# Block sums by kind, and the transposes of x2 moved between outputs, at the start of the second mixture of experts

## The reference

```python
x = attention(q, k, v)              # 2 x 8 heads x 768 x 64, banded mask
...                                 # as rows: N = 1536 tokens, D = 512
# second layer: hard routing over 8 experts, with a skip
y[mask] = gate_w[mask, None] * (np.maximum(xc[mask] @ w1[e], 0.0) @ w2[e])
x2 = x + y
# third layer: every token through all 4 experts, F = 1024
p = domain_probs / (domain_probs.sum(-1, keepdims=True) + 1e-09)
for e in range(4):
    h = np.maximum(x2 @ w1[e], 0.0)
    out += p[:, e:e + 1] * (h @ w2[e])
```

## Time and profile before

| what | us |
|---|---|
| median of 3 runs | 790.16 |
| the three runs | 790.33, 777.43, 790.16 |
| the profiled execution, its own time | 778.11 |
| span of its trace | 776.4 |
| PE busy in it | 743.0 |
| first product of the third layer starts at | 267.3 |
| second step starts at | 308.5 |

### The profile page before, as it was taken

The page is one execution under the profiler, slowest core; times in us unless marked ns, Lnnn a source line. Parts: engine busy times, 40 slices in busy tenths (PEclk is TensorE's granted clock), DMA queues, the critical chain, the costliest instruction groups (busy, mean ns, idle before and its releaser), DMA issues.

```text
span 776.4 us, 11260 instructions
## 1 busy us (share of the span) xinstructions
PE 743.0 (96%) x4199; PEld 661.5 (85%) x4199; DVE 471.6 (61%) x924; ACT 329.1 (42%) x586; POOL 42.2 (5%) x86
## 2 busy tenths in 40 slices
PE   3999999699999879999999999999999999999998
PEld 2889889488888778998989989989889899898896
DVE  5766666699888587654573475275365265456442
ACT  2666566388988352521432333234144043143230
POOL 3100100110100410000000000000000000000000
PEclk9999999699999999999999999999999999999999
DMA  9569970599990530030021011002003003000112
GB/s 152 101 152 247 291 217 21 199 394 390 390 389 35 156 130 1 1 109 1 0 71 39 1 55 54 1 17 92 0 0 108 0 0 109 0 0 0 41 41 81
DMA packets 86944, 79.28 MB, mean 102 GB/s; under 512 B 50802, under 2 KB 56948, under 8 KB 86900
## 3 DMA queue, kind: packets, MB, share of 16 engines
q1 hardware_dynamic: 81540, 71.32, 29.6%
q0 software_dynamic: 1600, 5.24, 2.2%
q10 hardware_dynamic: 3760, 2.14, 0.9%
HBM read 70.30 MB, written 8.39 MB: 101 GB/s over the span
## 4 chain that ended last, share of the span: by engine, by line
PE 89%; DVE 6%; DMA 2%; issue 1%; ACT 1%; POOL 0%; DVEq 0%; SPq 0%; POOLq 0%
PE ps L1881 32%; PE ps L1858 30%; PE ps L1761 11%; PE ps L1585 3%; PE ps L1610 2%; PE ps L1609 2%; PE ps L1594 2%; PE ps L1565 2%; PE ps L1626 1%; PE ps L1618 1%; PE ps L1736 1%; DVE xs L1448 1%; DVE X L1105 1%; PE ps L1817 1%; DVE ql L1065 1%
## 5 line engine op out<-in xcount | busy, mean ns | idle before, releaser
L1858 PE MATMUL ps<-xs,w1s 128*128 128x384 f32 x1344 | 237.7, 336 | 0.0
L1881 PE MATMUL ps<-w2s,h_hi 128*128 128x512 f32 x768 | 237.1, 390 | 0.6 <-DVE X L1486 0.6
L1858 PEld LDWEIGHTS ps<-xs,w1s 128*128 128x128 f32 x1344 | 235.1, 189 | 1.3
L1881 PEld LDWEIGHTS ps<-w2s,h_hi 128*128 128x128 f32 x768 | 143.7, 188 | 30.2 <-DVE X L1486 1.0
L1881 PE MATMUL ps<-w2s,h_lo 128*128 128x512 f32 x384 | 149.7, 390 | 0.0
L1488 DVE SCALAR_TENSOR_TENSOR X<-ps,prn,X 128x512 f32<-128x512 f32 x84 | 63.1, 751 | 121.7 <-PE ps L1881 121.3
L953 ACT ACTIVATE shared<-ps 128x384 f32<-128x384 f32 x96 | 46.1, 488 | 157.5 <-PE ps L1858 157.3
L1457 DVE TENSOR_TENSOR shared<-ps,shared 128x384 f32<-128x384 f32 x96 | 53.4, 557 | 93.6 <-PE ps L1858 93.3
L1881 PEld LDWEIGHTS ps<-w2s,h_lo 128*128 128x128 f32 x384 | 72.1, 188 | 15.0
L956 ACT ACTIVATE h_hi<-shared 128x384 fp32r<-128x384 f32 x96 | 50.5, 527 | 67.7 <-DVE shared L1457 67.7
L1023 DVE TENSOR_TENSOR piece_lo<-ring,piece_hi 128x1024 fp32r<-128x1024 f32 x48 | 56.4, 1220 | 5.4 <-ACT piece_hi L775 5.4
(11 more groups left out here) (183 smaller groups left out, 798.3 us busy)
## 6 DMA issues: line engine op xcount, KB each, us to landing
ring<-in_moe_w SPq DMA_DIRECT2D x24, 1024.0 KB, 12.3
raw<-in_moe_w SPq DMA_DIRECT2D x16, 1024.0 KB, 5.1
shared<-in_moe_w SPq DMA_DIRECT2D x8, 1024.0 KB, 10.7
X<-in_k SPq DMA_DIRECT2D x16, 192.0 KB, 4.3
shared<-in_q SPq DMA_DIRECT2D x16, 192.0 KB, 4.3
X<-in_v SPq DMA_DIRECT2D x16, 192.0 KB, 3.1
x_d<-X SPq DMA_DIRECT2D x8, 384.0 KB, 3.2
X<-x_d SPq DMA_DIRECT2D x2, 1536.0 KB, 16.5
```

What stands on the lines that cost most here:

```text
L1858: mm = pe.matmul(out_, w1s[:, wp, WI[name], c, f * P:(f + 1) * P], xs[:, 3 * b:3 * b + 3, xp, XI[name], c, :], start=(not onto and x == 0 ...
L1881: mm = pe.matmul(ps[:, 6 + k % 2, :], h_, w2s[:, wp, c, :], start=(x == 0 and c == 0), stop=(x == 2 and c == 3))
```

## The change

Four things change, and what is computed stays the same.

1. **Sums by kind.** For pairs 0 to 2 the sums are split in three kinds instead of all four at once: kind 0 is s3 (for P7), kind 1 is s1 and s2 (for P5 and P6), kind 2 is s4 (for P3). Each kind has a semaphore of its own for the high and the low part, and each product waits for its own kind.
2. **Order of the products.** P4 comes ahead of P6, in all 16 steps. ACT and DVE take the items in the new places (`copy(8, ...)`, `add(6, ...)`), in the same order as before.
3. **Transposes of pairs 3 to 5.** None is left among the products. Pair 3, 4 and 5 are transposed behind the outputs of tiles 0, 1 and 2, in other banks, and the DVE work on them is spread between the outputs.
4. **w2 of the first unit.** `w2_high` and `w2_low` move from the first step to the front, ahead of the work on pair 0. ACT waits there for `x2_begun`, which PE sets when it has transposed the first tile.

```diff
-        PAIR_BANK = ((4, 1), (5, 2), (6, 7), (6, 7), (1, 2), (4, 5))
+        PAIR_BANK = ((4, 1), (5, 2), (6, 7), (1, 4), (2, 5), (1, 4))
+        KIND = ((5, 6), (3, 5), (6, 7))
+        KIND_OF = {"P7": 0, "P6": 1, "P5": 1, "P3": 2}
-        ITEMS = [(p, f) for p in ("P1", "P2", "P7", "P6", "P4", "P5", "P3") for f in range(2)]
+        ITEMS = [(p, f) for p in ("P1", "P2", "P7", "P4", "P6", "P5", "P3") for f in range(2)]
...
+            def kind_high(g, p):
+                i, j = KIND[g]
+                if g < 2:
+                    act.wait_ge(s_step, 3 * p + (1, 3)[g])
+                else:
+                    act.wait_ge(s_made, p + 1)
+                act.activation(xs[:, p, 0, i:j, :, :].rearrange("p a k c -> p (a k c)"),
+                               xs_f[:, p, 1, i:j, :].rearrange("p a c -> p (a c)"), ACT.Copy).then_inc(kind_hi[g], 1)
...
                 for f in range(2):
                     copy(0, 0, f)
+                if begin:
+                    for f in range(2):
+                        copy(4, 1, f)
...
-                if inserted:
-                    inserted()
-                for f in range(2):
-                    copy(4, 1, f)
+                if begin:
+                    kind_high(2, 1)
+                    kind_high(2, 2)
+                else:
+                    for f in range(2):
+                        copy(4, 1, f)
...
-                    copy(6, 0, f)
+                    copy(8, 0, f)
...
+            act.wait_ge(x2_begun, 1)
+            for j in range(2):
+                w2_high(0, 0, j)
...
+            def kind_low(g, p):
+                i, j = KIND[g]
+                dve.wait_ge(kind_hi[g], p + 1)
...
-                    add(8, 0, f, 4)
+                    add(6, 0, f, 4)
...
             dve.wait_ge(x_ld, 32)
+            for j in range(2):
+                w2_low(0, 0, j)
             x2_low(0)
             s_sums(0)
             x2_low(1)
             x2_low(2)
             s_sums(1)
-            s_low(0)
-            s_sums(2)
-            s_low(1)
-            s_low(2)
-            x2_sum(6)
-            x2_sum(7)
+            s_sum(2, 0)
+            for p in range(3):
+                kind_low(0, p)
+            s_sum(2, 1)
+            s_sum(2, 2)
+            s_sum(2, 3)
+            for p in range(3):
+                kind_low(1, p)
...
             def x2_transposed(p):
-                pe.wait_ge(s_made, 3)
+                if p == 5:
+                    pe.wait_ge(s_made, 4)
+                else:
+                    pe.wait_ge(added, 2 * (p - 2))
...
-                    if begin and b == 0 and (name, f) == ("P2", 1):
-                        x2_transposed(3)
...
-                    if begin and k < 2:
-                        pe.wait_ge(added, 6)
-                        x2_transposed(4 + k)
+                    if begin and k < 3:
+                        x2_transposed(3 + k)
```

More of the change, by code:

```diff
@@ L404, in build @@
         s_made = sem("s_made")
+        x2_begun = sem("x2_begun")
         s_hi = sem("s_hi")
         s_lo = sem("s_lo")
+        kind_hi = [sem(f"kind_hi{g}") for g in range(3)]
+        kind_lo = [sem(f"kind_lo{g}") for g in range(3)]
         raw1_ld = sem("raw1_ld")
@@ L983, in m2_units @@
                     begin = first and not half
-                    for j in range(2):
-                        w2_high(m, half, j)
                     if begin:
-                        step(m, half, 0, lambda: x2_high(3))
+                        step(m, half, 0, True)
+                        x2_high(3)
+                        x2_high(4)
                         s_high(3)
-                        x2_high(4)
                         x2_high(5)
@@ new lines, in s_sums @@
+            def s_sums(p):
+                for i in range(4):
+                    s_sum(p, i)
+            def kind_low(g, p):
+                i, j = KIND[g]
+                dve.wait_ge(kind_hi[g], p + 1)
+                if g:
+                    dve.wait_ge(s_made, p + 1)
+                here = xs_f[:, p, 1, i:j, :].rearrange("p a c -> p (a c)")
+                dve.tensor_tensor(xs[:, p, 1, i:j, :, :].rearrange("p a k c -> p (a k c)"), here,
+                                  xs[:, p, 0, i:j, :, :].rearrange("p a k c -> p (a k c)").bitcast(F32), ALU.subtract).then_inc(kind_lo[g], 1)
@@ L1493, in m2_units, with middle @@
                     if begin:
[L1494 to L1498, removed]
+                        def middle():
+                            for p in range(3):
+                                kind_low(2, p)
                         step(m, half, 0, middle)
-                        for k in range(8, NT):
-                            x2_sum(k)
-                        s_low(3)
+                        x2_sum(6)
+                        x2_sum(7)
                         outputs(m, half, 0, 0, True)
+                        x2_sum(8)
+                        x2_sum(9)
+                        x2_low(3)
+                        outputs(m, half, 0, 1, True)
+                        s_sums(3)
+                        x2_sum(10)
+                        x2_sum(11)
+                        outputs(m, half, 0, 2, True)
                         x2_low(4)
                         s_sums(4)
-                        outputs(m, half, 0, 1, True)
+                        outputs(m, half, 0, 3, True)
                         x2_low(5)
                         s_sums(5)
+                        outputs(m, half, 0, 4, True)
+                        s_low(3)
                         s_low(4)
-                        outputs(m, half, 0, 2, True)
+                        outputs(m, half, 0, 5, True)
                         s_low(5)
-                        for k in range(3, 6):
-                            outputs(m, half, 0, k, True)
                     else:
@@ L1868, in outputs @@
                     if begin and k < 2:
[L1869 removed]
+                        pe.wait_ge(s_made, 3)
                     else:
```

58 lines of the change are left out of this document (37 added, 21 removed).

## The result

| | median, us | runs |
|---|---|---|
| before | 779.3 | 777.43, 778.1, 779.3, 790.16, 790.33 |
| changed | 773.41 | 773.04 to 773.99, 5 runs |

The changed kernel takes 0.9934 of the time before, 95% interval 0.9924 to 0.9945: 0.66% or 5.1 us less, the sign and nearly the size forecast. The predicted 783.8 us is 10.4 us too high, and lies even above the 779.3 us measured for the kernel before, because the median that it started from, 790.16, belongs to a group of rarer times of the same kernel, which the ratios leave out with few exceptions.

A forecast was written before the change was run, and what follows sets the result against it. PE bounds the kernel, busy 743.0 of 776.4 us; its first step would fall from 41.2 to 34.3 us, 6.9 less, minus 0.6 for gathers: 790.16 - 6.3 = 783.8 us, 8-in-10 range 769.5 to 788.

The forecast's parts named there:

- the new wait: First step, P4: PE waits 0.6 us for ACT's copy of P7, bounds 0 and 2 us, replacing the 4.68.
- the wait of 0.56: First step's outputs, at 302.93: PE's idle time of 0.56 us goes, since outputs come ahead of the long splits.
- DVE's last split: End of first step: DVE's split of the last sums ends at 304.5, with 1.7 us to spare before second-step P7.
- carry the difference over: Base of the forecast: median 790.16 lies 12 us above the profiled execution; subtracting 6.3 from it gives 783.8 us.
- 0.3 for each of two gathers: First gathers, beside DVE's early split of w2: delayed 0.6 us in all, bounds 0 and 2.1 us.
- the row of 1.25: Second layer's gather at 209.18, under a DVE split: took 1.25 us, used as the typical price for the first gathers.
- 18.9 us forecast: First step's outputs: 16.4 us of output matmuls, 2.4 of three transpose blocks, 0.1 allowed for waits.
- The full hold of 2.1 us: First gathers: rival that they are held up by 2.1 us, saving 4.8, time 785.4 us; chance 0.12.
- P4 late in every step: Seventh item of 15 other steps: rival that P4 waits for P7's copy; at 1 us each 798.9 us; chance 0.04.
- comes back at P4: P4 or second step: rival that the wait returns, 2 us more, saving 3 to 4.5, 785.7 to 787.2 us; chance 0.14.
- something else than splits and tile sums set the 4.68 us: PE's stop ahead of P7: rival that banks or gathers set it, saving near 0, time 790 us; chance 0.02.
- Within 2%: Whole kernel: change in time under 2% (15.8 us), called about what a measurement can tell; chance 0.85.

The follow-up runs named there:

- e_after_again: The changed kernel unaltered, run again beside the variant with both improvements: 0.9950 of the time before, stretch 52.42 us against 51.47 in its first profile.
- e_copies_early: Changed kernel, but ACT makes the two copies of P1 ahead of its split of s1 and s2 of pair 2: 0.9912 of the time before, stretch 50.95 us.
- e_held_long: Kernel with the late split of w2, plus one unused 128x2048 DVE difference over the first gather: one run, 774.95 us, stretch 53.93 us.
- e_copy_thrice: Changed kernel with two unused extra ACT copies of P7's first half ahead of the counted one in 15 later steps: 1.0069 of the time before.
- each half alone: Changed kernel with all four sums split at once (0.9982 of the time before), or with pair 3 transposed ahead of P7 again (0.9989).
- e_w2late: Changed kernel with the split of the first unit's w2 back in the first step: 0.9918 of the time before, stretch 52.53 us.
- e_p6first: Changed kernel with the old order of products, P6 ahead of P4, in all 16 steps: 0.9927 of the time before, stretch 51.36 us.

## Why the prediction was right and wrong

**Right: the mechanism and its place.** P7 waited for nothing (for 0.43 us in e_after_again), 84 matmuls ran at a granted clock of 1.00 in 15.54 us (15.4 forecast), and the new wait stood at P4, for ACT's copy, with 0.58 us (0.6 forecast; 0.77 in e_after_again). e_copies_early showed that it is the copies of P1 ahead of it. Three blocks of 0.79 us of transposes run between outputs, the wait of 0.56 is gone, DVE's last split comes 2.0 us ahead of its need (1.7 forecast, counted to P7's start and not to its third pass, which reads it), and the later steps take the same time.

**Wrong: the base of the forecast.** The step that failed is the sentence "No row tells what the 12 us are, so I carry the difference over: 790.16 - 6.3". Two of three runs shown were at 790, and I took the median for the kernel's level. With five runs it is 779.3, and of the 56 runs of the kernel before, 8 were near 790, one at 787.2. That two of the first three were among them was bad luck; to take their median for the level was the error. The profiled execution, whose rows all the terms came from, was the better base: 778.11 - 6.3 = 771.8, 1.6 us from the median measured. The last section shows where 12 us arise in two executions of variants of the changed kernel; no execution of the kernel before with a time near 790 was profiled, so for it this is inferred.

**Mis-sized: the gathers.** The term "0.3 for each of two gathers" measured 0.88 on the first and nothing on the second; the first product came 0.75 us later against the transposes (16.79 instead of 16.04). The bounds of 0 and 2.1 held it. I took the row of 1.25 as a typical price, though each of the rows has its own cause: how much of DVE's instruction is left when the gather is issued. With e_held_long this is shown. That the rows near 1.25 speak against a lock was a misreading: the one at 209.18 ends 0.82 us behind the DVE instruction that was in progress, as the last section shows.

**Mis-sized: the outputs.** 18.9 us forecast (16.4 + 2.4 + 0.1), 19.14 measured: 12 output matmuls take 2.72 to 2.76 us from start to start, but 2.85 or 2.86 right behind a block of transposes, and I had booked 0.1 in all for this. The products took 0.14 more than forecast. With 0.15 more for the gathers this makes the stretch 5.77 instead of 6.3 us shorter.

**The rivals.** The full hold of 2.1 us did not come, because the gather got through between DVE's two instructions. P4 late in every step did not come: 467.9 and 468.0 us, and e_copy_thrice gives the price if it had. The 2 us more of the wait that "comes back at P4" did not come. That something else than splits and tile sums set the 4.68 us falls too: the stop is gone, and each half alone shortens it, to 3.31 and 2.05 us.

**Chances.** Within 2% was right. But 0.66% stands clear of the noise of this kernel, and I had called 2% about what a measurement can tell: the interval of this one reaches 0.1% to either side.

## What to carry to other kernels

When an engine waits for the last of a queue of steps, list all that stand ahead of it on the engine it waits for: here two different groups of steps had to go, and each alone gave a seventh or a quarter of the saving (a third or a half, if the gathers ahead of it are left out). Work that is moved into idle time of one engine has to be checked against what the others do in that time, above all a gather that the path depends on. And a saving is subtracted from the execution whose rows it was read from; when the runs shown lie in two groups, the level of the median is a question of its own.

## What the runs showed of the hardware

**A gather issued by POOL waits for the DVE instruction in progress.** In each case the gather's row ends 0.82 to 0.83 us behind the end of a DVE instruction that reads two operands from SBUF and writes to SBUF: 256.15 + 1.22 = 257.37, and 256.36 + 1.83 = 258.19; 257.57 and 258.40 in e_held_long; 208.39 + 1.22 = 209.61, and 210.43. In the pair at 288.30 and 288.39 it is the first of two scalar-tensor-tensor instructions of 0.74 us (289.04 and 289.86). In the twelve traces 105 gathers took over 1 us, and all of them end 0.81 to 0.84 us behind such an instruction; the 135 others took 0.94 or 0.95 us, most with DVE idle or reading PSUM. The row of 3.07 is a gather that missed the gap between two such instructions (173.28) and ends behind the second (172.06 + 2.35 = 174.41, and 175.23), the 1.83 one got in. It is the same gather in every trace (3.06 to 3.08 us); why it misses the gap isn't shown. The Trainium skill, "SBUF — State Buffer", section "SBUF: two separate sides", says that the port pair which DVE and GpSimd share is an exclusive lock for a whole instruction, also for a DVE operation with two SBUF inputs against a GpSimd operation that reads SBUF. For GpSimd's side the traces agree, with the rows near 1.25 too, which the prediction had counted against it. DVE is not seen to wait for a gather: its second instruction ran on while the gather's last 0.82 us passed, and the two took 2.35 us, as at 281.56 without a gather.

**PE at little more than half its rate with a granted clock of 1.00.** The profiled executions of e_w2late and e_p6first took 785.52 and 784.59 us, against 772.1 to 774.9 in the lower group. The stretch from 28 to 40 us, in attention, before, and in e_p6first:

```profile
28.00:40.00 12.00, 11.79 (x109) 10.64 (x108) 8.78 (x34) 7.69 (x20) 1.66 (x4) 1.00 0.25 56
...
28.00:40.00 12.00, 12.00 (x62) 11.08 (x62) 5.11 (x19) 4.45 (x10) 0.00 (x0) 1.00 0.07 17
```

PE is busy throughout in both and does 109 matmuls in one and 62 in the other. This goes on until about 50 us, and from there on the kernel is some 11.9 us late (first transposes of x2 at 263.18 instead of 251.26) and loses no more.

The lower rate is not peculiar to these two. From 16 to 22 us each of six traces looked at has 28 or 29 matmuls, and what differs is when the rate rises. From 22 to 28 us, before, changed, and e_p6first:

```profile
22.00:28.00 6.00, 6.00 (x47) 5.54 (x46) 4.86 (x18) 3.55 (x9) 0.84 (x3) 1.00 0.87 161
...
22.00:28.00 6.00, 6.00 (x38) 5.46 (x36) 4.07 (x13) 3.05 (x7) 0.86 (x3) 1.00 0.67 136
...
22.00:28.00 6.00, 6.00 (x32) 5.66 (x30) 4.23 (x14) 3.05 (x7) 1.01 (x3) 1.00 0.75 133
```

It rises at about 24 us before and at about 26 in the changed kernel, and this is 1.0 of the 1.1 us between the starts of their stretches; in e_p6first and e_w2late it rises near 50. The column of the granted clock shows 1.00 in all these rows, so it doesn't tell this; the count of matmuls in a busy stretch does. All this is long before the change. Times of the upper group occur in both kernels, but only variants of the changed one were profiled in it. Why the rate rises late in some executions isn't known; nothing was tried on it.
